# Two steps of a level in one half slot: a new order of attention steps beside a matmul stream

## The reference

```python
B, H, S, D = 4, 8, 768, 48
f = 1 / (1 + exp(-f_logit))
for t in range(S):
    state = f[:, :, t, :, None] * state + einsum('bhd,bhe->bhde', k[:, :, t], v[:, :, t])
    y[:, :, t] = einsum('bhd,bhde->bhe', q[:, :, t], state)
x = y.transpose(0, 2, 1, 3).reshape(B * S, H * D)         # 3072 x 384
h = x @ w_in                                              # 384 -> 2048
g = where(h >= 1, h, where(h <= -1, 0, (h + 1) ** 2 / 4))
x1 = g @ w_out                                            # 2048 -> 384
gate = x1 @ w_gate                                        # 384 -> 1536
out = (gate * sigmoid(gate) * (x1 @ w_val)) @ w2_out      # 1536 -> 384
```

## Time and profile before

| | |
|---|---|
| median of 3 runs | 1100.32 us (1100.22 to 1100.85) |
| profiled execution | 1098.95 us, span 1097.1 us |
| mean granted PE clock | 0.971 |
| busy share of the span | PE 93%, PEld 76%, DVE 52%, ACT 41%, POOL 38% |
| prologue (attention of unit 0) | 24 to 81 us |
| stage one with attention beside it | 81 to about 560 us |
| stage one, last unit, and stage two | from there to the end |

### The profile page before, as it was taken

The page is one execution under the profiler, slowest core; times in us unless marked ns, Lnnn a source line. Parts: engine busy times, 40 slices in busy tenths (PEclk is TensorE's granted clock), DMA queues, the critical chain, the costliest instruction groups (busy, mean ns, idle before and its releaser), DMA issues.

```text
span 1097.1 us, 19162 instructions
## 1 busy us (share of the span) xinstructions
PE 1018.2 (93%) x7816; PEld 830.3 (76%) x7816; DVE 572.0 (52%) x823; ACT 454.1 (41%) x840; POOL 415.1 (38%) x288
## 2 busy tenths in 40 slices
PE   1564999999999999999999999999999999999998
PEld 1463778778777876877788888888888888888886
DVE  3974995896599389749944642323222222222221
ACT  6447546653754664385525532222222122222221
POOL 1665773554365255336525622121212222221211
PEclk9676999999999999999999999999999999999999
DMA  9314003201400510040043101010010010000000
GB/s 359 146 55 158 1 2 125 117 1 40 173 30 2 164 78 2 3 153 30 2 153 135 58 1 58 1 58 1 1 58 1 1 58 1 30 1 1 29 1 29
DMA packets 17366, 63.51 MB, mean 58 GB/s; under 512 B 1920, under 2 KB 2176, under 8 KB 16512
## 3 DMA queue, kind: packets, MB, share of 16 engines
q1 hardware_dynamic: 17280, 62.30, 15.7%
HBM read 52.85 MB, written 9.44 MB: 57 GB/s over the span
## 4 chain that ended last, share of the span: by engine, by line
PE 82%; DVE 9%; issue 5%; ACT 3%; POOL 2%; DMA 0%; POOLq 0%; DVEq 0%; ACTq 0%; SPq 0%
PE acc L447 10%; PE acc L448 9%; PE acc L449 9%; PE bank L474 7%; PE bank L473 7%; PE bank L475 7%; PE hid L433 6%; PE bank L346 5%; PE hid L434 5%; PE hid L435 5%; DVE scores L746 4%; PE hid L474 2%; PE hid L475 2%; PE hid L473 2%; DVE queries L731 2%
## 5 line engine op out<-in xcount | busy, mean ns | idle before, releaser
L929 POOL TENSOR_TENSOR g_lo<-prod,g_hi 128x512 fp32r<-128x512 f32 x72 | 93.0, 1292 | 347.5 <-ACT g_hi L652 347.5
L922 POOL TENSOR_TENSOR g_lo<-act_tmp,g_hi 128x512 fp32r<-128x512 f32 x96 | 133.0, 1385 | 207.5 <-ACT g_hi L613 207.3
L837 DVE TENSOR_TENSOR sig<-sig,bank 128x512 f32<-128x512 f32 x72 | 49.5, 688 | 275.5 <-ACT sig L646 275.5
L892 POOL TENSOR_TENSOR keys<-keys,gates 128x512 f32<-128x512 f32 x82 | 123.4, 1505 | 92.8 <-PE bank L346 52.7
L652 ACT CAST g_hi<-prod 128x512 fp32r<-128x512 f32 x72 | 44.8, 622 | 247.8 <-PE acc L449 247.8
L433 PE MATMUL hid<-x_hi,win_hi 128*128 128x512 f32 x288 | 120.5, 418 | 24.1 <-DVE act_tmp L825 24.1
L746 DVE COPY_PREDICATED scores<-mask,bank 64x512 f32<-64x512 int32 x144 | 133.9, 930 | 12.7 <-PE bank L346 10.9
L613 ACT CAST g_hi<-act_tmp 128x512 fp32r<-128x512 f32 x96 | 59.5, 620 | 180.6 <-DVE act_tmp L825 180.6
L346 PEld LDWEIGHTS bank<-right_q,keys 128*64 128x64 f32 x2304 | 81.8, 151 | 62.4 <-issue 58.9
L346 PE MATMUL bank<-right_q,keys 128*64 128x64 f32 x2304 | 91.8, 239 | 39.4 <-ACT right_q L548 32.1
L447 PE MATMUL acc<-g_hi,wout_hi 128*128 128x512 f32 x288 | 117.2, 407 | 3.4 <-POOL g_lo L922 3.4
(11 more groups left out here) (79 smaller groups left out, 1876.5 us busy)
## 6 DMA issues: line engine op xcount, KB each, us to landing
gates<-in_f_dram SPq DMA_DIRECT2D x12, 512.0 KB, 5.2
queries<-in_q_dram SPq DMA_DIRECT2D x12, 512.0 KB, 4.9
keys<-in_k_dram SPq DMA_DIRECT2D x12, 512.0 KB, 4.7
values<-in_v_tok_dram SPq DMA_DIRECT2D x6, 1024.0 KB, 8.1
q_tok<-in_q_tok_dram SPq DMA_DIRECT2D x12, 384.0 KB, 9.0
k_tok<-in_k_tok_dram SPq DMA_DIRECT2D x12, 384.0 KB, 9.4
x_dram<-x_out SPq DMA_DIRECT2D x6, 768.0 KB, 3.4
x_raw<-x_dram SPq DMA_DIRECT2D x6, 768.0 KB, 5.6
```

The lines of the kernel that those rows point to most:

```text
L892: pool.tensor_tensor(kl, kl, right.broadcast_to([P, BP // 2 * P // (2 * m), m]), ALU.mult).then_inc(k_scaled, 1)
L922: pool.tensor_tensor(g_lo[:, c % RING, :], act_tmp[:, 2 + c % 2, :], g_hi[:, c % RING, :].bitcast(F32), ALU.subtract).then_inc(g_lo_done, 1)
```

## The change

The 14 half slots of the steps are set anew. The two steps of a level get the same half slot and stand right behind each other on every engine; the next level comes two or three half slots later. The levels end at half slot 17 instead of 19. Nothing else is altered.

```diff
 H_SIGMOID = (-2, -1)
 H_GATED = (-1, 0)
-H_STEP = (1, 3, 5, 7, 8, 9, 10, 12, 13, 14, 15, 17, 18, 19)
+H_STEP = (1, 1, 4, 4, 7, 7, 9, 9, 12, 12, 14, 14, 17, 17)
 H_LAST_MERGE = 21
 H_Y = (21, 21, 22, 22)
```

## The result

The changed kernel takes 1125.01 us (median of 4 runs, 1124.36 to 1126.75) against 1100.27 us of the kernel before in the same comparison: a ratio of 1.0227, 95% interval 1.021 to 1.0243. The forecast was 1128 us, the range 1106 to 1142. The profiled execution took 1124.36 us, its span is 1122.6 us, 25.5 us more than before.

The account below looks back on a forecast made before the run. PE was taken as the bound, with DVE a few microseconds behind in the level phase. 4 x 6.8 us (units 2 to 5) + 2 (unit 1) + 0 (prologue) gave +29 on 1098.95 us: 1128 us, range 1106 to 1142.

Parts of the forecast that it names:

- Every second M: Sign on DVE: every second merge should take 1.0 to 1.5 us, its first only 0.2 to 0.7.
- part 4: DVE's work ahead of `activate(4)`, from the first scaling: 38.3 us instead of 31.0, so it ends 7.2 us later.
- three K waits: On DVE, second merges wait for POOL's `keys` scaling: 1.25, 1.1 and 1.0 us for runs of 2, 4 and 8.
- a sign against itself: The forecast would be wrong if DVE showed gaps ahead of `activate(4)`.
- part 1: On PE, pairing saves 0.2 us of entering and leaving per pair, 7 us; the second level's bank is long free.
- The stalls spread: Rival: PE also waits at a pair's second level, two slow-clock stretches, +3 us per unit, 1141 us; chance 0.15.
- part 6: Granted clock falls once per unit behind the longest stall, adding 1.5 us: 6.8 us per unit.
- part 7: Unit 1: hidden(5) some 5 us late, partly offset by other gains; +2 us at the outputs, bounds -1 and +5.
- part 8: Prologue: waits for POOL's `keys` scaling replace weight-split waits; outputs start at 70.8 us; 0 taken, bounds -3 and +3.
- no port wait: Rival: DVE keeps the SBUF port through a pair's merges and scalings; +14, 1114 us; chance 0.22.
- The rival that pairs pay off: Rival: PE saves 7 us of switching and the present stalls vanish; -18, 1082 us; chance 0.09.

Follow-up runs that it names:

- run 2: Not a follow-up kernel: the level that works on runs of 2, in the changed kernel as in the kernel before; no measured time of its own.
- e_stagger: Level starts of the changed kernel, but each second step one half slot later, so no pairs: 1096.85 us, 0.9974 of the kernel before.
- small K: POOL's `scale_k` cut to one eighth of its elements: 1103.04 us in the changed kernel, 1091.42 us in the kernel before.
- late_pairs_early: Staggered steps up to step 7, then the last three levels paired at half slots 12, 14 and 17 as in the changed kernel: 1110.60 us.
- take_between: Changed kernel with the take of a pair's second step put off to the next level, between first scaling and second merge: 1110.12 us.
- one_pair_undone: Changed kernel with only the pair of steps 6 and 7 taken apart, step 7 going from half slot 9 to 11: 1119.36 us.
- late_pairs: Staggered steps up to step 7, then the last three levels paired at half slots 13, 15 and 17: 1118.25 us, ratio 1.0165.
- take_behind: Changed kernel with the take of a pair's second step put off to the next level, behind both scalings: 1120.57 us, ratio 1.019.

## Why the prediction was right, point by point

- **The mechanism held.** The wait `hid L433 <- act_tmp L825` grew from 24.1 to 45.5 us (forecast 45 to 50), with 0.94 us ahead of hidden(2), 3.7 us ahead of hidden(6) and 1.8 around hidden(5) (forecast 1, 4 and 2); 3.50 us of the total are a stall in unit 1 that was not forecast. The second merges of runs of 4 and 8 took 1.71 and 1.38 us (forecast 1.0 to 1.5), first ones 0.63 and 0.43. "Every second M" was too wide: in unit 2 these two of six were long, in unit 1 four of six, in the prologue all six.
- **DVE's sum ahead of `activate(4)` (part 4)**: 38.3 us forecast, 37.3 measured. Two of the three K waits came as priced: 1.71 - 0.63 = 1.1 and 1.38 - 0.43 = 0.95 (forecast 1.1 and 1.0). The first did not come as a merge's wait: K of run 2 started later, and it was the second scaling (1.98 us instead of 0.69) that waited for it. One gap came that the forecast had at nothing, and had named as a sign against itself: 0.73 us at 215.25, where DVE's scaling waits for ACT's copy. The old order had two gaps in this place, of 0.69 and 0.78 us, where the takes wait for PE. Over the run DVE's waits for that copy grew from 0.2 to 11.8 us (17 times), with the full K and the small one alike, and are 0.3 us without pairs (e_stagger); most of them stand behind the long stall. No run took them away by themselves, so their share in the rest that does not hang on K is not shown.
- **The bank (part 1)** was not "long free". A level uses the bank of the take three steps back; the second level of steps 6 and 7 waited 0.78 us for it in each of units 2 to 5, and such waits made 7.9 us in all. They stand ahead of a later wait for `activate` and so, as the rival *The stalls spread* argued against itself, they are covered.
- **PE's saving (part 1)** was undersized. The pair at 206.03 has its 64 instructions in 2.08 us, and the next matmul starts 2.01 us behind its start:

```profile
206.03 2.08 PE L346 MATMUL bank<-right_q,keys 128*64 128x64 f32 x64
208.04 0.50 PE L433 MATMUL hid<-x_hi,win_hi 128*128 128x512 f32 x1
```

  Alone, a level had 1.08 us there; so the second one costs 0.93 against 1.30, 0.37 us saved per pair instead of 0.2. PE's busy time fell by 1.5 us only, because the granted clock fell from 0.971 to 0.963 on the mean; over the span that is some 10 us of slower work by an estimate (if PE was busy while it was slow), so that PE's work without it fell by some 11 us where 7 was forecast. PE could not use it, as it waits for DVE.
- **The clock (part 6)** was taken as one fall per unit. Two stretches of the changed kernel (columns as above):

```profile
243.00:247.00 4.00, 3.78 (x9) 2.63 (x9) 2.60 (x7) 3.63 (x6) 1.29 (x1) 0.57 0.00 0
```

```profile
441.00:449.00 8.00, 5.99 (x18) 4.43 (x18) 7.29 (x10) 1.22 (x2) 4.58 (x3) 0.79 0.00 1
449.00:452.00 3.00, 2.82 (x27) 2.16 (x29) 1.83 (x5) 2.79 (x5) 1.29 (x1) 1.00 0.00 0
```

  In units 2, 3 and 5 it fell behind the long stall and cost its time. In unit 4 it fell one stall earlier, ahead of the 2.18 us wait, where PE waits for DVE anyway: the stall is 1.5 us shorter by it and the unit loses nothing by the clock. And the kernel before had its own 2.21 us stall with a slow clock in just this unit, which I had not taken off: before, unit 4 was 2.6 us longer than unit 3. That is why unit 4 lost only 1.3 us where +6.8 was forecast; units 2, 3 and 5 lost 5.3 to 5.5.
- **Unit 1 (part 7)** is the term that was wrong: +2 forecast, bounds -1 to +5, measured +7.3. The stall at hidden(5) came (4.63 us), 21.8 us of DVE behind S0 where 22.2 was forecast. A second of 3.50 us at 161.89 followed, since the late levels have no more room than the early ones; that sentence of mine was an estimate without a row. POOL has the `wout` splits here as well (the scaling at 136.36, beside one of them, took 2.10 us), and unlike in units 2 to 5 the later second merges too waited for K:

```profile
138.38 1.36 DVE L720 TENSOR_TENSOR gates<-gates 128x128 f32<-128x128 f32 x1
...
148.10 1.18 DVE L720 TENSOR_TENSOR gates<-gates 128x64 f32<-128x64 f32 x1
...
156.26 1.10 DVE L720 TENSOR_TENSOR gates<-gates 128x32 f32<-128x32 f32 x1
```

  The granted clock was 0.50 behind the first stall (126 to 130 us) and 0.62 behind the second (162 to 166), where the forecast had one slow stretch. With the small K the second stall shrinks to 0.50 us and the unit loses 1.4 us instead of 7.3. late_pairs_early shows the second stall too (2.41 us at 159.38), e_stagger only 0.80 us.
- **The prologue (part 8)**: 71.7 against 70.8 forecast and 71.0 before. The part's own terms (-1.1 + 6.1 - 4 or 5) add up to 0 to +1, not to 70.8. The exchange of split waits for K waits was as described (the six second merges took 5.9 us more than the first ones, 6.1 forecast), and take_between showed the exchange from the other side.
- **The sum**: 27.2 + 2 + 0 forecast, 17.5 + 7.3 + 0.7 measured. Units 2 to 5 were too high by 10 us, unit 1 too low by 5. That the 1128 is nearer to 1125 than its parts are is luck.
- **The split of the cause** came out of the runs: about half of the loss goes with K's length, the other half stays with a small K, and in unit 2 it stands as DVE's work ahead of `activate(4)` (two takes, a scaling and a merge more). In "no port wait" I had that at 14 of 29; the run with a small K has 11.6.
- **The rival that pairs pay off** is out for every placing that was tried: seven pairs dense (1125), seven at the old pace (1112.5), six (1119), three late ones (1118 and 1111).

## What to carry to other kernels

Before two steps are set side by side on one engine, write down what stands between them today and what runs on the other engines under it: here a take of 1.5 to 2.7 us was the only cover for POOL's scaling, and every way of removing it cost 10 us or more. A stall that is missing in a trace says nothing about a place where the engine arrives late because of an earlier stall. Taking away the last of several stalls (one_pair_undone) can leave most of the loss, while moving one small step from ahead of the first late wait, where there is only one, gave 0.7%.

## What the runs showed of the hardware

In the rows read here, a DVE instruction with two SBUF inputs and a POOL instruction that met did not get on together, whichever came first; the later one ended roughly its own length after the other. A short one pays most: a merge of 16 elements took 1.04 us instead of 0.18, because it waits for the whole K of 1.50 us (late_pairs). Takes that read PSUM kept their time: 1.43 to 1.50 us for two beside a K in the kernel before, 1.39 to 1.44 with no POOL instruction beside them in take_behind. When both wait for the same merge, DVE's scaling goes first and K is longer by 0.6 to 0.7 us (1.70 and 1.83 against 1.12 us). When DVE's next merge follows a scaling without a gap and K has been waiting, POOL is ahead of it (K at 228.37, merge at 228.89, 1.71 us). That no row of before had shown.

The lower clock level following a stall is not a price in itself. In one_pair_undone the granted clock behind a 2.86 us wait was 0.50 for four microseconds, and the time was lost. In unit 4 of the changed kernel it fell behind a 1.04 us wait (0.79 on eight microseconds) and cost next to nothing, since the next wait was 1.5 us shorter. Nor does the length of the wait alone say whether it falls: behind the 1.03 us wait of unit 2 it stayed at 1.00 (235 to 243 us), and so it did behind a 2.93 us wait in unit 4 of one_pair_undone (436 to 440 us). What else decides it is not shown by these runs.
